# The joint splits with k above q: ScalarE places q's lower part, DMAs copy q's upper part and double k in another order, early loads spread to one a head

## What is computed

```python
# q, k, v: (4, 8, 576, 64)
scores = scale * np.matmul(q, k.transpose(0, 1, 3, 2))      # scale = 1/8
mask = block_i >= block_j                                   # blocks of 64
scores = np.where(mask, scores, -1000000000.0)
attn = np.exp(scores - max); attn = attn / (sum + 1e-09)
x = np.matmul(attn, v)                                      # -> (2304, 512)
h = x @ w_in;  g = h * np.clip(h + 3.0, 0.0, 6.0) / 6.0;  x = g @ w_out
h = x @ w_in2; g = h * np.tanh(log1p(exp(h)));            out = g @ w_out2
```

## Time and profile before

| | |
|---|---|
| Time, median of 3 runs | 992.28 us (992.13 to 992.98) |
| The profiled execution's own time | 989.68 us |
| Its span | 987.9 us |
| PE busy | 950.5 us (96% of the span) |
| DVE busy | 755.1 us (76%) |
| ACT busy | 648.3 us (66%) |
| POOL busy | 417.4 us (42%) |
| Mean granted TensorE clock | 0.997 of full speed |
| DMA, mean over the span | 219 GB/s |
| Chain that ended last | PE 76%, DMA 7%, DVE 6%, SP's queue 5% |

### The profile page before, as it was taken

One profiled execution on the slowest core, in us unless ns is written; L12 is line 12 of the kernel. 1 busy time (PEld: TensorE's weight loads), 2 busy tenths in 40 slices (PEclk: granted clock), 3 DMA queues, 4 the chain that ended last, 5 costly groups with the idle time before them and its releaser, 6 DMA issues.

```text
span 987.9 us, 17731 instructions
## 1 busy us (share of the span) xinstructions
PE 950.5 (96%) x6004; PEld 847.5 (86%) x6004; DVE 755.1 (76%) x1435; ACT 648.3 (66%) x1426; POOL 417.4 (42%) x393
## 2 busy tenths in 40 slices
PE   6897998999999999998999999999999999999998
PEld 5786887899888888887888889898899898988896
DVE  6787998878686765879797786876877877777654
ACT  7787998865455454544446556777777777776663
POOL 6676776467766585968686680000000000000000
PEclk9999999999999999999999999999999999999999
DMA  6778887764788978587977545646645655465255
GB/s 187 221 215 253 243 228 211 204 190 143 226 285 301 315 256 279 187 301 263 314 245 257 203 154 187 224 156 227 225 171 208 229 180 194 172 232 203 90 191 191
DMA packets 86329, 216.43 MB, mean 219 GB/s; under 512 B 10720, under 2 KB 17504, under 8 KB 86240
## 3 DMA queue, kind: packets, MB, share of 16 engines
q1 hardware_dynamic: 86096, 215.01, 65.6%
q10 hardware_dynamic: 144, 0.29, 0.1%
HBM read 162.07 MB, written 39.92 MB: 204 GB/s over the span
## 4 chain that ended last, share of the span: by engine, by line
PE 76%; DMA 7%; DVE 6%; SPq 5%; issue 2%; POOL 1%; ACT 1%; ACTq 0%; DVEq 0%; POOLq 0%
PE psum L1004 36%; PE psum L887 11%; PE psum L889 11%; PE psum L888 11%; DMA klo<-klo 5%; PE psum L833 3%; PE psum L812 2%; DMA ext_d<-ext_made 2%; PE psum L792 1%; SPq L548 1%; DVE ebuf L1565 1%; DVE xlo L1500 1%; DVE glo L1571 1%; PE psum L793 1%; DVE ostage L1407 1%
## 5 line engine op out<-in xcount | busy, mean ns | idle before, releaser
L1004 PE MATMUL psum<-ghi,osplit 128*128 128x512 f32 (+1 forms) x640 | 215.9, 371 | 0.3 <-POOL osplit L1846 0.3
L887 PE MATMUL psum<-xhi,whi 128*128 128x256 f32 (+1 forms) x640 | 187.3, 293 | 2.8 <-ACT snap L1209 2.6
L889 PE MATMUL psum<-xhi,wlo 128*128 128x256 f32 (+1 forms) x640 | 186.8, 292 | 0.0
L888 PE MATMUL psum<-xlo,whi 128*128 128x256 f32 (+1 forms) x640 | 186.6, 292 | 0.0
L1004 PE MATMUL psum<-osplit,ghi 128*128 128x512 f32 x576 | 180.7, 395 | 1.3 <-DVE glo L1571 1.3
L1571 DVE SCALAR_TENSOR_TENSOR glo<-ebuf,ghi 128x512 fp32r<-128x512 f32 x144 | 126.3, 877 | 25.7 <-ACT ghi L1257 17.7
L887 PEld LDWEIGHTS psum<-xhi,whi 128*128 128x128 f32 x640 | 120.8, 189 | 15.7 <-ACT snap L1209 3.8
L1846 POOL TENSOR_TENSOR osplit<-oraw,osplit 128x512 fp32r<-128x512 f32 x80 | 116.1, 1454 | 38.3 <-ACT osplit L1176 34.2
L1004 PEld LDWEIGHTS psum<-ghi,osplit 128*128 128x128 f32 x640 | 117.9, 189 | 16.3 <-issue 0.5
L1257 ACT ACTIVATE ghi<-ebuf 128x512 fp32r<-128x512 f32 x144 | 90.2, 627 | 62.4 <-DVE ebuf L1565 34.3
L888 PEld LDWEIGHTS psum<-xlo,whi 128*128 128x128 f32 x640 | 120.8, 189 | 10.7
(11 more groups left out here) (113 smaller groups left out, 2137.9 us busy)
## 6 DMA issues: line engine op xcount, KB each, us to landing
ext<-ext_d SPq DMA_DIRECT2D x56, 768.0 KB, 4.4
osplit<-o_d SPq DMA_DIRECT2D x80, 512.0 KB, 5.3
oraw<-in_w_out SPq DMA_DIRECT2D x80, 256.0 KB, 5.7
wraw<-in_w_in SPq DMA_DIRECT2D x32, 512.0 KB, 5.2
ext_d<-ext_made SPq DMA_DIRECT2D x32, 384.0 KB, 5.3
attn_t<-ostage SPq DMA_DIRECT2D x64, 144.0 KB, 2.5
qkin<-in_qk SPq DMA_DIRECT2D x30, 288.0 KB, 3.5
o_d<-staged SPq DMA_DIRECT2D x32, 256.0 KB, 5.3
```

Source lines behind the costliest of these rows:

```text
L887: pe.matmul(dst, hi, xh, start=(start and cc == 0), stop=False, skip_group_check=True)
L888: pe.matmul(dst, hi, xl, start=False, stop=False, skip_group_check=True)
L889: last = pe.matmul(dst, lo, xh, start=False, stop=(stop and cc == 1), skip_group_check=True)
L1004: last = pe.matmul(bank(Y_BANK + c, n), stat, mov, start=(first and m == 0), stop=(final and m == 2), skip_group_check=True)
```

## The change

The rows of q and k in `qkin` are exchanged: k in rows 0 to 63, q in rows 64 to 127. So POOL's joint split leaves q's parts in the lower halves of `khi` and `klo`. q's low part then stands in the rows in which `qs` needs it, and ACT copies it there (`place_q_lo`, 64x576); q's high part stands in the wrong rows, and a DMA moves it up (`move_q_hi`), after which `move_k_hi` may write over it; `move_k_lo` may write over q's low part once ACT has placed it. ACT no longer rounds q from `qkin`. There are still three moves of 144 KB a head. `place_q_lo` stands in ACT's step behind `exps(n, 4)`, where `split_q_hi` stood at the step's end. The early loads and POOL's early jobs move to later steps, and x's four chunks go to four steps in place of two. The splits of heads 0 and 1 are the same work as before.

```diff
-EARLY_JOBS = {2: 0, 5: 1, 8: 2, 11: 3}
+EARLY_JOBS = {3: 0, 6: 1, 9: 2, 12: 3}
-EARLY_X_LOAD, NEXT_X_LOAD = {9: (0, 1), 10: (2, 3)}, (27, 29)
-EARLY_X_ADD, EARLY_X_SCALE, EARLY_X_MIX = (14, 15, 16, 17), (15, 16, 17, 18), 19
-EARLY_X_HI, EARLY_X_LO = (20, 21, 22), (21, 22, 23)
-EARLY_LOADS = {0: 0, 2: 1, 5: 2, 8: 3, 11: 4, 14: 5}
+EARLY_X_LOAD, NEXT_X_LOAD = {10: (0,), 11: (1,), 13: (2,), 14: (3,)}, (27, 29)
+EARLY_X_ADD, EARLY_X_SCALE, EARLY_X_MIX = (15, 16, 17, 18), (16, 17, 18, 19), 20
+EARLY_X_HI, EARLY_X_LO = (21, 22, 23), (22, 23, 24)
+EARLY_LOADS = {0: 0, 2: 1, 6: 2, 9: 3, 12: 4, 15: 5}
...
                     sp.wait_ge(qk_lo, n - QK - DIRECT + 1)
-                    sp.wait_ge(q_hi, n - QK + 1)
...
-            def move_q_lo(n):
-                sp.wait_ge(qk_lo, n - DIRECT + 1)
+            def move_q_hi(n):
+                sp.wait_ge(qk_hi, n - DIRECT + 1)
+                s = n % QK
+                sp.dma_start(qs[s][0:DH, 0:SEQ].bitcast(F32), khi[s][DH:P, :].bitcast(F32)
+                             ).then_inc(q_hi_moved[s], 16)
+
+            def move_k_hi(n):
                 s = n % QK
-                sp.dma_start(qs[s][DH:P, 0:SEQ].bitcast(F32), klo[s][0:DH, :].bitcast(F32)
-                             ).then_inc(q_lo_moved[s], 16)
-
-            def move_k_hi(n):
-                sp.wait_ge(qk_lo, n - DIRECT + 1)
+                sp.wait_ge(qk_lo, n - DIRECT + 1)
+                sp.wait_ge(q_hi_moved[s], moves(n))
+                sp.dma_start(khi[s][DH:P, :].bitcast(F32), khi[s][0:DH, :].bitcast(F32)
+                             ).then_inc(k_hi_moved[s], 16)
+
+            def move_k_lo(n):
+                sp.wait_ge(q_lo_ready, n - DIRECT + 1)
...
+            move_q_hi(DIRECT)
             for n in range(FIRST, NHEAD):
                 if QK <= n + 6 < NHEAD:
                     load_qk(n + 6)
-                if 2 <= n + 3 < NHEAD:
-                    load_v(n + 3)
+                if DIRECT <= n + 3 < NHEAD:
+                    move_k_lo(n + 3)
+                    move_k_hi(n + 3)
...
                 if n in NEXT_X_LOAD:
...
-                if DIRECT <= n + 3 < NHEAD:
-                    move_k_lo(n + 3)
+                if DIRECT < n + 4 < NHEAD:
+                    move_q_hi(n + 4)
+                if 2 <= n + 3 < NHEAD:
+                    load_v(n + 3)
                 if in_use(n) and n != LAST:
                     store_o(n)
-                if DIRECT <= n + 4 < NHEAD:
-                    move_q_lo(n + 4)
-                    move_k_hi(n + 4)
...
                 elif i == 0:
-                    pe.wait_ge(q_hi, n + 1)
-                    pe.wait_ge(q_lo_moved[n % QK], moves(n))
+                    pe.wait_ge(q_lo_ready, n - DIRECT + 1)
...
+            def place_q_lo(n):
+
+                act.wait_ge(qk_lo, n - DIRECT + 1)
+                nc.scalar.activation(qs[n % QK][DH:P, 0:SEQ], klo[n % QK][DH:P, :].bitcast(F32), ACT.Copy
+                                     ).then_inc(q_lo_ready, 1)
...
                     exps(n, 4)
+                if in_use(n) and in_use(n + 3):
+                    place_q_lo(n + 3)
                 if in_use(n + 1):
                     exps(n + 1, 0)
-                if in_use(n + 1):
                     exps(n + 1, 1)
+                if n + 3 == DIRECT:
+                    place_q_lo(DIRECT)
...
-                if n == -1:
-                    split_q_hi(2)
-                if in_use(n + 4) and n >= -1:
-                    split_q_hi(n + 4)
```

More of the change, by code:

```diff
@@ L332, in build @@
         qk_lo = sem("qk_lo")
-        q_lo_moved = [sem(f"q_lo_moved{s}") for s in range(QK)]
+        q_lo_ready = sem("q_lo_ready")
+        q_hi_moved = [sem(f"q_hi_moved{s}") for s in range(QK)]
         k_hi_moved = [sem(f"k_hi_moved{s}") for s in range(QK)]
@@ L517, in load_qk @@
                     sp.wait_ge(qk_lo, n - QK - DIRECT + 1)
-                    sp.wait_ge(q_hi, n - QK + 1)
                 sp.dma_start(qkin[n % QK][:, :], qk[n, :, :]).then_inc(qk_loaded[n % QK], 16)
-            def move_q_lo(n):
-                sp.wait_ge(qk_lo, n - DIRECT + 1)
-                s = n % QK
-                sp.dma_start(qs[s][DH:P, 0:SEQ].bitcast(F32), klo[s][0:DH, :].bitcast(F32)
-                             ).then_inc(q_lo_moved[s], 16)
-            def move_k_hi(n):
-                sp.wait_ge(qk_lo, n - DIRECT + 1)
-                s = n % QK
-                sp.dma_start(khi[s][0:DH, :].bitcast(F32), khi[s][DH:P, :].bitcast(F32)
+            def move_q_hi(n):
[4 more added lines that the diff above has]
+            def move_k_hi(n):
+                s = n % QK
+                sp.wait_ge(qk_lo, n - DIRECT + 1)
+                sp.wait_ge(q_hi_moved[s], moves(n))
+                sp.dma_start(khi[s][DH:P, :].bitcast(F32), khi[s][0:DH, :].bitcast(F32)
                              ).then_inc(k_hi_moved[s], 16)
             def move_k_lo(n):
+                sp.wait_ge(q_lo_ready, n - DIRECT + 1)
                 s = n % QK
-                sp.wait_ge(q_lo_moved[s], moves(n))
-                sp.dma_start(klo[s][0:DH, :].bitcast(F32), klo[s][DH:P, :].bitcast(F32)
+                sp.dma_start(klo[s][DH:P, :].bitcast(F32), klo[s][0:DH, :].bitcast(F32)
                              ).then_inc(k_lo_moved[s], 16)
@@ L687, in store_y @@
                     sp.dma_start(dst, src).then_inc(y_stored[c], 16)
-            sp.dma_start(ostage[0][:, :], qk_first[0, 1, :, :]).then_inc(k_loaded[0], 16)
+            sp.dma_start(ostage[0][:, :], qk_first[0, 0, :, :]).then_inc(k_loaded[0], 16)
             load_qk(2)
-            sp.dma_start(qkin[1][:, :], qk_first[1, 0, :, :]).then_inc(qk_loaded[1], 16)
-            sp.dma_start(ostage[1][:, :], qk_first[1, 1, :, :]).then_inc(k_loaded[1], 16)
+            sp.dma_start(qkin[1][:, :], qk_first[1, 1, :, :]).then_inc(qk_loaded[1], 16)
+            sp.dma_start(ostage[1][:, :], qk_first[1, 0, :, :]).then_inc(k_loaded[1], 16)
             load_v(0)
             load_v(1)
+            move_q_hi(DIRECT)
             for n in range(FIRST, NHEAD):
@@ L1057, in _ @@
         def _(act):
-            act.dma_start(qkin[0][:, :], qk_first[0, 0, :, :]).then_inc(qk_loaded[0], 16)
+            act.dma_start(qkin[0][:, :], qk_first[0, 1, :, :]).then_inc(qk_loaded[0], 16)
             act.preload_act_table_set("natural_log_exp_and_others")
             def split_q_hi(n):
[L1063 to L1067, removed]
+                act.wait_ge(qk_loaded[n], 16)
+                nc.scalar.activation(qs[n][:, 0:SEQ], qkin[n][:, :], ACT.Copy).then_inc(q_hi, 1)
+            def place_q_lo(n):
+                act.wait_ge(qk_lo, n - DIRECT + 1)
+                nc.scalar.activation(qs[n % QK][DH:P, 0:SEQ], klo[n % QK][DH:P, :].bitcast(F32), ACT.Copy
+                                     ).then_inc(q_lo_ready, 1)
             def split_second_k_hi():
@@ L1911 @@
     nc = bacc.Bacc("TRN2", target_bir_lowering=False, num_devices=1, dynamic_dma_scratch_size=2048)
-    qk = np.stack([heads(q).transpose(0, 2, 1), heads(k).transpose(0, 2, 1)], axis=1)
+    qk = np.stack([heads(k).transpose(0, 2, 1), heads(q).transpose(0, 2, 1)], axis=1)
     v_rows = np.pad(heads(v), ((0, 0), (0, PADSEQ - SEQ), (0, 0)))
```

## The result

| | before | changed |
|---|---|---|
| Median | 992.13 us (989.97 to 992.98, 7 runs) | 986.16 us (983.64 to 988.46, 7 runs) |
| The profiled execution's own time | 989.68 us | 986.87 us |
| Its span | 987.9 us | 985.1 us |

The ratio is 0.9943, 95% interval 0.9927 to 0.9959: 6 us faster where 14.5 were forecast, outside the range of 969 to 985. Faster it is, by 0.4 to 0.6 of what was forecast.

A forecast was written before the change was run, and what follows sets the result against it. PE in the head loop was taken to be held by a loop of PE, DVE, SP and DMA, k's low part landing last. 24.9 - 1.6 - 2.5 - 3.6 - 0.4 - 2.3 = 14.5 us gained: 977.8 us, range 969 to 985.

The forecast's parts named there:

- The Trainium skill's fit for the GpSimd path: DMA time as fixed 2.0 us plus bytes over 436 GB/s: 2.3 us per 144 KB move, no queue; sum 23.3 us.
- Early jobs a step later cost nothing.: Early-job tables: moving them later costs 0, since the first feed-forward step comes 7 heads and more after the last.
- head 19 at 5.37 + 2.3 us: Step 15, weight load and sums' store both ahead of k's high part: landed at T + 9.35, 2.3 us late.
- slower: ACT held by POOL: Rival, chance 0.05: ACT's copy waits for POOL's low part mid-step in every head; 13.9 us slower, 1006.2 us.
- The term for weight loads: k's high part behind a weight load: issued T + 2.8, landing 4.7 us, 0.5 us late; five heads, 2.5 us.
- less to spare than forecast: Ordinary heads: k's high part issued 2.1 us after the head's store (T), landing 3.3 us, 1.6 us to spare.
- The term for x chunks: k's high part behind an x chunk: issued T + 3.9, landing 4.0 us, 0.9 us late; four heads, 3.6 us.
- q's move landed long before.: SP's order: move_k_hi also waits for q's move, issued one step earlier and landed long before; no cost given.
- The most there is to gain: Head loop: 29 heads at 5.37 us would save 23.9 us, plus 1.04 ahead of head 2: 24.9 us.
- the forecast had 17.13: Start of the head loop: 1.04 us to gain ahead of head 2, whose first score matmul stood at 18.17.
- 1.6 for POOL: ACT's copy waits for POOL's split behind a weight job in steps 3, 6, 9, 12: 0.4 us each, 1.6 us.
- The rival of k's high part as the new last wait: Rival, chance 0.14: landing of 5.2 us becomes the rule, PE's wait moves to k's high part; 981.3 us.

The follow-up runs named there:

- e1: The changed kernel with POOL's early work on x (add, scale, mix, splits) two steps later: 985.35 us, ratio 0.9909 of the kernel before.
- e3: The kernel before with the new step tables alone: 998.39 us, ratio 1.0032.
- e8: e5 with the early loads spread over more steps, the last x chunk again one step before POOL's first add: 983.81 us, ratio 0.9898.
- e6: e1 with the early loads cut to a sixteenth of their columns, a measure of time alone: 979.97 us, ratio 0.9854.
- e4: e1 with k's two moves ahead of the load of qkin on SP, sums' store and early loads behind them: 982.46 us, ratio 0.9883.
- e11: e5 with the store of a head moved behind k's two moves: 996.47 us, ratio 1.0021.
- e5: e4 with the sums' store and early loads behind q's move and the load of v, ahead of the next store: 977.43 us, ratio 0.9846.
- e2: The changed layout, copy and DMA order with the step tables of before: 989.0 us, ratio 0.9949.
- e12: The changed kernel itself, timed once more against the kernel before: 986.95 us, ratio 0.9918.

## Why the prediction was wrong, point by point

**Right.** PE's wait on k's low part, held in a loop with SP's store, is what the change takes away; ordinary heads take 5.32 to 5.45 us, so ACT's copy costs next to nothing where it stands; what remains, beside the stop, is a wait for k's high part behind loads. The stages behind attention hardly changed (791.2 us from head 31 to the end, before 790.1). The Trainium skill's fit for the GpSimd path ("DMA: Bandwidth & Descriptors", Anatomy of one DMA), 2.3 us for such a move as an estimate, agrees with the least landing of a move into `khi` or out of it in this trace (2.3) and lies far under the median of 4.1.

**"Early jobs a step later cost nothing."** This step failed. I looked at how long after them the first feed-forward step comes, and not at the distance between the last x load and the first add, which the same tables cut from four steps to one. The forecast had head 19 at 5.37 + 2.3 us, and it took 10.9: 3.2 us missing. The rival "slower: ACT held by POOL" had the path, ACT's copy waiting for POOL in the middle of its step, but for every head and not for what stood ahead of POOL's split in one. e1 takes the stop away and leaves 7.63 us; e3 and e8 bring it about in other kernels.

**The term for weight loads, 0.5 us on each of five heads.** This is the largest miss. The five heads took 8.3 us more than 5.37 each, not 2.5; 7.0 us of it are waits for k's high part. The landing was 5.30 to 6.33 us, not 4.7: I had capped it by the longest of the kernel before (5.2), where one move stood behind the loads and not two. The clock has no part in it: the granted clock read 1.00 in all five. Nor is it mainly the weight's 512 KB that makes the landing long, as I had it (5.40 and 5.79 us with 32 KB, e6). Ordinary heads had less to spare than forecast as well: in step 5 k's high part was issued at T + 2.35 (46.66 to 49.01), not T + 2.1, and its median landing was 4.3 us, not 3.3, which leaves 0.35 us and not 1.6. The term for x chunks held: 3.0 us measured, 3.6 forecast (T + 2.1 + 1.70 is T + 3.8 and not T + 3.9, which would make it 3.2).

**"q's move landed long before."** Not behind loads: it took 4.44 us to land at head 16, and SP stood 0.46 us for it. I had given it no term. In e4 and e11 SP stood 2.2 and 2.4 us.

**The most there is to gain, 24.9 us.** Too high. I took 5.37 us for every head, but DVE's three reciprocals of 0.94 us lengthen heads 11, 19 and 27 (5.55 to 6.13 us even where nothing waits, as in e5), and ACT's splits of x, one of 0.62 us in each of three heads, lengthen heads 25 and 26 (5.82 and 5.87 us): some 3 us that none of these orders of DMAs gave back. ACT was nearly as full as PE (161.50 and 167.16 of 180 us).

**The start.** Head 2 began at 18.57, where the forecast had 17.13. No wait is in it; matmuls ran slow until 19.9, 0.59 us at 17.15 against 0.38 at 23.62 for the same form. In e2 and e4 the same head starts at 17.2 and 17.3, in e1 and e5 at 18.8 and 18.6, in e12 at 18.66. The durations are those of the lower level of the clock, but the granted clock of the profile reads 1.00 from 14 to 20 us, so the cause of these 1.4 us stays open.

Summed for the profiled execution, against the forecast's head 31 at 183.3: start 1.4, weights 5.8, stop 3.2, reciprocal and x splits 1.5, head 3 0.5, less 0.6 for x chunks and 1.6 for POOL, which was not seen (head 7, behind a weight job alone, took 5.32 us): 10.2 of the 10.6 us missing. This accounts for the one profiled execution, in which less was gained than between the medians. The rival of k's high part as the new last wait (981.3) was the closest of the cases, and it too lacked the stop.

## What to carry to other kernels

A table that moves a load and its user moves two ends of one interval: look at the distance between them on each queue, above all where the user stands ahead of work that others need. And in a queue that issues in order, look at what stands just ahead of a transfer that is waited for: with k's moves ahead of the load of `qkin`, and the early loads behind q's move, the same bytes gave 0.9846 in place of 0.9909.

## What was not expected of the hardware

The median landing of the 144 KB move of k's high part inside SBUF rose from 2.5 us to 4.3, and that of k's low part from 3.3 to 4.3, with the mean DMA share going only from 0.78 to 0.83. The longest, 6.3 us, came behind loads of 512 KB and 288 KB; with the early loads cut to a sixteenth the same move still took 5.8, and the median of k's high part 3.9. In e4, where k's two moves stood ahead of the 288 KB, it was 2.6. One wait of PE of 2.63 us was followed by 5 us at a granted clock of 0.50, while the waits of up to 1.67 us in the same trace left it at 1.00. The matmuls of the first heads become fast some 1.4 us earlier in some profiles than in others, with a granted clock of 1.00 in all of them, and nothing here shows why.
